# Linear attention in chunks of 64 tokens of two batches instead of 128 tokens of one

## The chip, the core and the metric

The kernel runs on one core of a Trainium2 chip. Five engines work side by side: TensorE (PE, with its weight loads shown apart as PEld), VectorE (DVE), ScalarE (ACT), GpSimd (POOL) and SyncE (SP), whose queue issues most of the transfers. They meet by semaphores only. The metric is the device time of one execution in microseconds (us), as the median of several runs.

## What is computed

Three layers follow one another: a linear attention with decay, a routed expert layer, and a dense layer with squared ReLU. The change touches only the first. In it, 4 batches of 8 heads with head dimension 48 run over 768 tokens; w (one decay per head and channel) scales the state from token to token, u weighs the token's own key and value.

```python
B, H, S, D = r.shape                       # 4, 8, 768, 48
for t in range(S):
    kt, vt, rt = (k[:, :, t], v[:, :, t], r[:, :, t])
    cur = np.einsum('bhd,bhe->bhde', u[None] * kt, vt)
    y[:, :, t] = np.einsum('bhd,bhde->bhe', rt, state + cur)
    state = w[None, :, :, None] * state + np.einsum('bhd,bhe->bhde', kt, vt)
```

The output rows (3072 tokens x 384) go to the router and the experts (`_moe_ref`), and then through `h = np.maximum(x @ w_in, 0.0)` and `(h * h) @ w_out` (`_moe2_ref`).

## The kernel before

The kernel is written out engine by engine; each engine's program order is fixed by hand, and semaphores release it.

**Units.** The attention is cut into 24 units (NU), six chunks of 128 tokens for each of four batches. Unit n = 4i + b is chunk i of batch b. Each batch has its own state tile, so a state that unit n leaves is needed again by unit n + 4. Heads go in four pairs (PAIRS): head a = 0 of a pair lies on partitions 0 to 47, head a = 1 on 64 to 111.

**One unit.** DVE scales keys and queries by powers of the decay (`scale`: `ks`, lines 710, and `rs`, 711). TensorE then runs these stages, of which each has a function:

- `scores` (L1166): 8 matmuls of keys against queries, weights 48 rows x 128 columns, 128 columns streamed, head 0 and head 1 by turns in the upper and lower rows of the array, into `sc_ps`, one bank for each.
- `inter` (L1179): 8 matmuls of queries against the state, weights 48 x 128, 128 columns streamed, into `y_ps`.
- `turn` (L1233): 3 transposes of the output rows of the unit before, 128 x 128.
- `back` (L1204): 16 matmuls of masked scores against values, weights 128 rows x 64 columns, 64 columns streamed, the two halves of the columns by turns, added to `y_ps`.
- `own_term` (L1220): 8 matmuls, weights 112 x 64, of which 2 columns are streamed (the term with u).
- `gate` (L1241): 6 matmuls, weights 128 x 64, 8 columns streamed (the router's logits of the unit before).
- `state_update` (L1192): 8 matmuls of scaled keys (`kn`) against values, weights 128 x 48, 48 columns streamed, into `u_ps`.

DVE masks the scores (`mask`, L717, two instructions of 128 x 512 from PSUM), adds the output's two parts (`rows`, L739) and updates the state (`state_sum`, L728, four instructions of 112 x 48). POOL makes `kn` (L426) and `rk` (L435) and splits a quarter of a dense weight tile (L441). ACT copies logits and transposed rows and scales values (L564). SP loads `tt` and `nn` four units ahead and stores the output rows (L334), one transfer of 128 rows for each unit.

**Order on TensorE.** In the loop's step for unit n it does scores(n+1), inter(n+1), turn(n-1), back(n), own_term(n+1), gate(n-1), state_update(n+1). DVE does mask(n+1), scale(n+2), rows(n), state_sum(n+1). `kn` and `u_ps` are single: `kn` of unit n+1 is made when state_update(n) is done, and `u_ps` is written again when state_sum(n) is done. The last chunk's units need no update; of them only unit 20 does one.

**Precision.** All matmuls of the attention are fp32. Each is recorded as two passes, with a weight load and a matmul for each pass; a transpose has one pass. So a stage of 8 matmuls has 16 records.

## Time and profile before

| | us |
|---|---|
| median of 3 runs | 809.96 |
| lowest, highest | 808.62, 810.9 |
| the profiled execution | 810.82 |
| its span in the trace | 809.1 |

The trace holds one execution. Its span begins with the first instruction and ends with the last; 1.7 us of the execution's own time lie around it. The attention fills the first 125 us or so, routing comes next, and the experts and the dense layer fill the rest. In the whole span PE is busy 775.9 us (96%), DVE 501.0 (62%), ACT 321.4 (40%), POOL 293.9 (36%). Starts of instructions are recorded; ends of matmuls are modelled, so lengths of stages are best read from one stage's start to the next one's.

### The profile page before, as it was taken

Reading aid. Unit: us, or ns where it says so; the run is one execution under the profiler, and the core shown is the slowest. Engines: PE = TensorE matmul, PEld = TensorE weight load, DVE = VectorE, ACT = ScalarE, POOL = GpSimd, SP = SyncE. Lnnn points to the kernel's source line nnn. Section 1 sums busy time; section 2 is a strip of 40 time slices with the busy share of each in tenths; the row PEclk is TensorE's granted clock in tenths of the full one; section 3 lists DMA queues with packets and bytes.
Section 4 is the critical chain, followed back from the end, with each engine's and each line's share of the span. In section 5 each row is a group of like instructions: output and inputs, shape, how many; then the busy total and the mean of one; then the engine's idle time right before and its main releaser. Section 6 shows DMA issues by size and latency. Waiting matters only on the chain.

```text
span 809.1 us, 19168 instructions
## 1 busy us (share of the span) xinstructions
PE 775.9 (96%) x6971; PEld 742.5 (92%) x6971; DVE 501.0 (62%) x1195; ACT 321.4 (40%) x718; POOL 293.9 (36%) x295
## 2 busy tenths in 40 slices
PE   8999994699999999999999999999999999999996
PEld 6999993589899999999999999999999999999995
DVE  7988886788846783678367836783778326721210
ACT  4566554314532354235323532353235324531432
POOL 7766640102631163116312631263126312621333
PEclk9999996799999999999999999999999999999998
DMA  8878744502300140014001400130013002300000
GB/s 225 260 236 244 240 122 176 184 2 79 108 1 30 35 149 0 29 42 142 0 29 49 135 0 29 52 133 0 29 59 126 0 30 79 108 1 30 0 1 30
DMA packets 22196, 65.27 MB, mean 81 GB/s; under 512 B 3664, under 2 KB 6736, under 8 KB 22160
## 3 DMA queue, kind: packets, MB, share of 16 engines
q1 hardware_dynamic: 19088, 55.34, 21.5%
q0 software_dynamic: 3072, 9.44, 3.3%
q8 instruction: 24, 0.39, 0.2%
q14 instruction: 12, 0.10, 0.0%
HBM read 55.33 MB, written 9.44 MB: 80 GB/s over the span
## 4 chain that ended last, share of the span: by engine, by line
PE 77%; DVE 12%; issue 5%; POOL 3%; ACT 1%; DMA 1%; POOLq 0%; DVEq 0%; SPq 0%; ACTq 0%
PE bank L1362 14%; PE bank L1372 13%; PE bank L1369 13%; PE bank L1429 6%; PE bank L1430 6%; PE bank L1431 6%; PE bank L1166 3%; PE bank L1204 3%; PE bank L1179 3%; DVE hot L977 2%; DVE sq L1076 2%; DVE w_lo L294 1%; PE bank L1233 1%; POOL xg L476 1%; PE bank L1220 1%
## 5 line engine op out<-in xcount | busy, mean ns | idle before, releaser
L503 POOL TENSOR_TENSOR h_lo<-sq,h_hi 128x384 fp32r<-128x384 f32 x128 | 155.4, 1217 | 376.2 <-DVE sq L1076 375.9
L1076 DVE SCALAR_TENSOR_TENSOR sq<-bank,relu 128x384 f32<-128x384 f32 x128 | 71.0, 555 | 150.7 <-ACT relu L627 148.7
L627 ACT ACTIVATE relu<-bank 128x384 f32<-128x384 f32 x128 | 62.8, 491 | 191.9 <-PE bank L1372 165.0
L1429 PE MATMUL bank<-m_hi,h_hi 128*128 128x384 f32 x384 | 132.5, 345 | 2.3 <-POOL h_lo L503 2.0
L1430 PE MATMUL bank<-m_lo,h_hi 128*128 128x384 f32 x384 | 130.0, 339 | 0.0
L1362 PE MATMUL bank<-x_hi,m_hi 128*128 128x384 f32 x384 | 129.6, 337 | 0.0
L1431 PE MATMUL bank<-m_hi,h_lo 128*128 128x384 f32 x384 | 129.6, 337 | 0.0
L1372 PE MATMUL bank<-x_hi,m_lo 128*128 128x384 f32 x360 | 121.6, 338 | 0.0
L1369 PE MATMUL bank<-x_lo,m_hi 128*128 128x384 f32 x360 | 121.0, 336 | 0.0
L621 ACT ACTIVATE h_hi<-bank 128x384 fp32r<-128x384 f32 x64 | 31.4, 491 | 175.3 <-PE bank L1372 149.4
L1068 DVE SCALAR_TENSOR_TENSOR h_lo<-bank,h_hi 128x384 fp32r<-128x384 f32 x64 | 35.5, 555 | 73.6 <-ACT h_hi L621 73.6
L1429 PEld LDWEIGHTS bank<-m_hi,h_hi 128*128 128x128 f32 x384 | 72.2, 188 | 4.5 <-POOL h_lo L503 4.5
L1362 PEld LDWEIGHTS bank<-x_hi,m_hi 128*128 128x128 f32 x384 | 72.4, 189 | 0.0
L1431 PEld LDWEIGHTS bank<-m_hi,h_lo 128*128 128x128 f32 x384 | 72.3, 188 | 0.0
L1430 PEld LDWEIGHTS bank<-m_lo,h_hi 128*128 128x128 f32 x384 | 72.3, 188 | 0.0
L629 ACT ACTIVATE h_hi<-relu 128x384 fp32r<-128x384 f32 x128 | 67.3, 526 | 4.1
L1372 PEld LDWEIGHTS bank<-x_hi,m_lo 128*128 128x128 f32 x360 | 67.9, 189 | 0.0
L1369 PEld LDWEIGHTS bank<-x_lo,m_hi 128*128 128x128 f32 x360 | 67.9, 189 | 0.0
L1362 PE MATMUL bank<-x_hi,w_hi 128*128 128x384 f32 x192 | 67.3, 351 | 0.0
L1362 PE MATMUL bank<-h_hi,w_hi 128*128 128x384 f32 x192 | 64.5, 336 | 1.9 <-DVE h_lo L1068 1.9
L294 DVE TENSOR_TENSOR w_lo<-w_raw,w_hi 128x1024 fp32r<-128x1024 f32 x48 | 63.9, 1335 | 2.1 <-ACT w_hi L597 2.1
L1372 PE MATMUL bank<-h_hi,w_lo 128*128 128x384 f32 x192 | 64.4, 336 | 0.0
(199 smaller groups left out, 1473.2 us busy)
## 6 DMA issues: line engine op xcount, KB each, us to landing
w_raw<-we_in SPq DMA_DIRECT2D x48, 512.0 KB
nn<-nn_in SPq DMA_DIRECT2D x24, 384.0 KB, 4.2
tt<-tt_in SPq DMA_DIRECT2D x44, 192.0 KB, 4.4
m_raw<-m_in SPq DMA_DIRECT2D x12, 512.0 KB, 6.4
x_rows<-yrow SPq DMA_DIRECT2D x24, 192.0 KB, 2.4
tt<-tt_in SPq DMA_DIRECT2D x4, 256.0 KB, 5.7
xg<-x_rows,perm_next POOLq DMA_INDIRECT x24, 5.1
out<-xg,perm_now POOLq DMA_INDIRECT x24, 2.6
```

Of the source, the lines that this page charges most:

```text
L294: eng.tensor_tensor(w_lo[:, cols], w_raw[j % W_SLOTS][:, :], w_hi[:, cols].bitcast(f32), ALU.subtract).then_inc(w_lo_ready, 1)
L503: pool.tensor_tensor(h_lo[g % 3][:, :], sq[g % 2][:, :], h_hi[g % 3][:, :].bitcast(f32), ALU.subtract).then_inc(lo2_ready, 1)
L627: act.activation(relu[:, :], h_ps[g % 3][:, 0:CAP], ACT.Relu).then_inc(relu_ready, 1)
L629: act.activation(h_hi[g % 3][:, :], relu[:, :], ACT.Square).then_inc(h_hi_ready, 1)
L1068: dve.scalar_tensor_tensor(out=h_lo[g % 3][:, :], in0=h_ps[g % 3][:, 0:CAP], scalar=0.0, in1=h_hi[g % 3][:, :].bitcast(f32), op0=ALU.max, ...
L1076: dve.scalar_tensor_tensor(out=sq[g % 2][:, :], in0=h_ps[g % 3][:, 0:CAP], scalar=0.0, in1=relu[:, :], op0=ALU.max, op1=ALU.mult).then_inc ...
L1362: pe.matmul(out, hi_w, hi_x, start=first, stop=False)
L1369: pe.matmul(out, hi_w, lo_x, start=False, stop=False)
L1372: return pe.matmul(out, lo_w, hi_x, start=False, stop=last)
L1429: pe.matmul(acc_ps[t][:, 0:DM], h_hi[r][:, s], m2_hi[:, c:c + DM], start=first, stop=False)
L1430: pe.matmul(acc_ps[t][:, 0:DM], h_hi[r][:, s], m2_lo[:, c:c + DM], start=False, stop=False)
L1431: last = pe.matmul(acc_ps[t][:, 0:DM], h_lo[r][:, s], m2_hi[:, c:c + DM], start=False, stop=end)
```

## The change

A unit becomes a chunk of 64 tokens of two batches: tokens 0 to 63 of a unit belong to the one batch (c = 0), 64 to 127 to the other (c = 1). There are still 24 units, now 12 chunks of 2 pairs of batches, and a state tile holds two batches side by side (112 x 2 x 48 x 4). A state that unit n leaves is needed again by unit n + 2. On the host the inputs are put into this order.

- `scores` and `inter` become 16 matmuls each, weights 48 x 64, 64 columns streamed, over all four 64x64 tiles of the array.
- `state_update` becomes 16 matmuls, weights 64 x 48, in two halves: `update_straight` (rows of batch c into the columns of head c) before `turn`, and `update_across` (the other two tiles), laid between the matmuls of `back`.
- `back` keeps 16 matmuls of 64 columns, with 64 rows in place of 128: only the two straight tiles.
- `mask` becomes one instruction of 128 x 512 for both heads; `state_sum` four of 112 x 96.
- The power tables have 64 columns in place of 128. ACT copies a corner of the causal mask early, and shifts half of the unit numbers late.
- The rows of a unit are stored by two transfers of 64 rows. Unit 21 does an update too.
- TensorE's waits for the stages now stand apart from the matmuls (`pe_held`), and `back` waits for `inter_done` and for `update_half` as well.

```diff
+C = 64
+NB = 2
@@
-                    sp.dma_start(x_d[bass.ds(i * P + b * S, P), :], yrow[b][:, :]).then_inc(y_stored[b], 16)
+                    for c in range(NB):
+                        sp.dma_start(x_d[bass.ds(i * P + b // NB * C + (b % NB * NB + c) * S, C), :],
+                                     yrow[b][c * C:(c + 1) * C, :]).then_inc(y_stored[b], 16)
@@ mask
-                for a in range(2):
-                    dve.tensor_tensor(am[b % 2][:, a, :].rearrange("p (c t) -> p c t", c=4),
-                                      sc_ps[a].rearrange("p (c t) -> p c t", c=4),
-                                      causal[:, :].unsqueeze(1).broadcast_to([P, 4, P]), ALU.mult).then_inc(masked, 1)
+                dve.tensor_tensor(am[b % 2][:, :, :, :], sc_ps.rearrange("p a (q t) -> p a q t", q=PAIRS),
+                                  causal[:, 0:C].unsqueeze(1).unsqueeze(2).broadcast_to([P, 2, PAIRS, C]), ALU.mult).then_inc(masked, 1)
@@ state_sum
-                    done = dve.scalar_tensor_tensor(out=state[b][:, c], in0=state[b][:, c], scalar=w_chunk[:, p:p + 1],
-                                                    in1=u_ps[0:HD, c], op0=ALU.mult, op1=ALU.add)
+                    done = dve.scalar_tensor_tensor(out=state[b % NB][:, :, c], in0=state[b % NB][:, :, c], scalar=w_chunk[:, p:p + 1],
+                                                    in1=u_ps[0:HD, :, c], op0=ALU.mult, op1=ALU.add)
@@ scores
-                        last = pe.matmul(sc_ps[a][:, p * P:(p + 1) * P], ks[rows, p, :], rs[j][rows, p, :], start=True, stop=True)
+                        for t in range(0, P, C):
+                            last = pe.matmul(sc_ps[t:t + C, a, p * C:(p + 1) * C], ks[rows, p, t:t + C], rs[j][rows, p, t:t + C],
+                                             start=True, stop=True)
@@ inter
-                        last = pe.matmul(y_ps[j][:, a, p * P:(p + 1) * P], rs[j][rows, p, :], state[b][rows, p * D:p * D + P],
-                                         start=p == 0, stop=False)
+                        for c in range(NB):
+                            t = slice(c * C, (c + 1) * C)
+                            last = pe.matmul(y_ps[j][t, a, p * P:p * P + C], rs[j][rows, p, t], state[b % NB][rows, c, p * D:p * D + C],
+                                             start=p == 0, stop=False)
@@ state_update
+            def update_tile(b, p, a, c):
+                h = slice((2 * p + a) * D, (2 * p + a + 1) * D)
+                t = slice(c * C, (c + 1) * C)
+                return pe.matmul(u_ps[a * HALF:a * HALF + D, c, p * D:(p + 1) * D], kn[t, h], nn[b][t, 0, h], start=True, stop=True)
+            def update_straight(i, b):
+                n = 4 * i + b
+                pe.wait_ge(kn_ready, n + 1)
+                if not is_first(n):
+                    pe.wait_ge(state_ready, n + B // NB)
+                pe.sem_inc(pe_held, 1)
+                for p in range(PAIRS):
+                    for c in range(NB):
+                        last = update_tile(b, p, c, c)
+                last.then_inc(update_half, 1)
+            def update_across(b, p):
+                for c in range(NB):
+                    last = update_tile(b, p, 1 - c, c)
+                return last
@@ back
+                def token_tile(p, a, c):
+                    t = slice(c * C, (c + 1) * C)
+                    at = (2 * p + a) * D
+                    return pe.matmul(y_ps[j][t, a, p * P:p * P + C], am[j][t, a, p, :],
+                                     nn[b][t, :, :].rearrange("p x f -> p (x f)")[:, at:at + C], start=False, stop=p == PAIRS - 1)
                 for p in range(PAIRS):
                     for a in range(2):
+                        if update is not None and a == 1:
+                            crossed = update_across(update[1], p)
+                            if p == PAIRS - 1:
+                                crossed.then_inc(update_ready, 1)
+                        for c in range(NB):
+                            last = token_tile(p, a, c)
@@ units of TensorE
+                    if more:
+                        update_straight(*one)
+                    turn(n - 1, (b - 1) % B)
+                    back(i, b, one if more else None)
```

TensorE's program in the steady part of the attention, before: one turn of the loop's stages, each row a line, what it writes and reads, the columns of the weights x the columns streamed, and the count.

```order
L1166 MATMUL bank<-rs,ks 128x128 x8
L1179 MATMUL bank<-state,rs 128x128 x8
L1233 MATMUL bank<-ident,yrow 128x128 x3
L1204 MATMUL bank<-nn,am 64x64 x16
L1220 MATMUL bank<-u_pair,rk 64x2 x8
L1241 MATMUL bank<-wg,yT 64x8 x6
L1192 MATMUL bank<-nn,kn 48x48 x8
```

TensorE's program at the same place after the change, from the end of one unit's `back` into the next unit's; L1184 is `scores`, L1201 `inter`, L1209 the update, L1294 `turn`, L1257 `back`, L1281 `own_term`, L1302 `gate`.

```order
L1209 MATMUL bank<-nn,kn 48x48 x2
L1257 MATMUL bank<-nn,am 64x64 x4
L1209 MATMUL bank<-nn,kn 48x48 x2
L1257 MATMUL bank<-nn,am 64x64 x2
L1281 MATMUL bank<-u_pair,rk 64x2 x8
L1302 MATMUL bank<-wg,yT 64x8 x6
L1184 MATMUL bank<-rs,ks 64x64 x16
L1201 MATMUL bank<-state,rs 64x64 x16
L1209 MATMUL bank<-nn,kn 48x48 x8
L1294 MATMUL bank<-ident,yrow 128x128 x3
L1257 MATMUL bank<-nn,am 64x64 x2
L1209 MATMUL bank<-nn,kn 48x48 x2
```

The update moved from the end of the unit to both sides of `turn`, and a unit has 81 matmuls where it had 57.

DVE's program in the loop, one unit, before and then after.

```order
L717 TENSOR_TENSOR am<-bank,causal 128x512 x2
L710 TENSOR_TENSOR ks<-tt,kpow 112x512
L711 TENSOR_TENSOR rs<-tt,powr 112x512
L739 TENSOR_TENSOR yrow<-bank,ownv 128x384
L728 SCALAR_TENSOR_TENSOR state<-state,w_chunk,bank 112x48 x4
```

After the change, the same place:

```order
L734 TENSOR_TENSOR am<-bank,causal 128x512
L728 TENSOR_TENSOR ks<-tt,kpow 112x512
L729 TENSOR_TENSOR rs<-tt,powr 112x512
L755 TENSOR_TENSOR yrow<-bank,ownv 128x384
L744 SCALAR_TENSOR_TENSOR state<-state,w_chunk,bank 112x2x48 x4
```

The order of DVE's steps stays; one mask instruction is gone, and the four of the state are twice as wide.

## Rows read from the trace of the kernel before

**Rows 1.** Busy time by engine, stretches of the attention; columns as in its first line.

```profile
core 0: us, PE busy (x) PEld busy (x) DVE busy (x) ACT busy (x) POOL busy (x), PEclk, DMA share, GB/s
20.00:40.00 20.00, 19.96 (x481) 18.49 (x480) 18.43 (x37) 11.87 (x46) 16.11 (x15) 1.00 0.85 258
...
80.00:100.00 20.00, 20.00 (x466) 18.49 (x462) 17.44 (x39) 12.53 (x50) 13.69 (x14) 1.00 0.79 236
20.00:108.00 88.00, 87.96 (x2083) 81.55 (x2084) 78.78 (x168) 52.25 (x207) 60.30 (x58) 1.00 0.81 242
```

**Rows 2.** Waits from 20 to 108 us, longest first.

```profile
engine line waited for: us in total, times, longest us
ACT own L552 <- PE bank L1241: 26.5, 19, 1.5
POOL kn L426 <- PE bank L1192: 23.3, 17, 1.9
...
DVE am L717 <- PE bank L1166: 5.2, 17, 0.3
PEld bank L1204 <- issue: 3.2, 19, 0.2
...
DVE state L728 <- PE bank L1192: 2.3, 4, 0.6
...
PEld bank L1166 <- DVE rs L711: 0.2, 1, 0.2
```

**Rows 3.** Timeline of TensorE, one unit: start, length, engine, line, operation, operands, weights, shape, records.

```profile
start us, us, engine line op out<-in xcount [idle before <-releaser]
...
93.34 1.16 PE L1166 MATMUL bank<-rs,ks 48*128 48x128 f32 x16
94.34 1.06 PE L1179 MATMUL bank<-state,rs 48*128 48x128 f32 x16
95.33 0.55 PE L1233 MATMUL bank<-ident,yrow 128*128 128x128 f32 x3
95.81 1.15 PE L1204 MATMUL bank<-nn,am 128*64 128x64 f32 x32
96.79 0.58 PE L1220 MATMUL bank<-u_pair,rk 112*64 112x2 f32 x16
97.23 0.50 PE L1241 MATMUL bank<-wg,yT 128*64 128x8 f32 x12
97.58 0.54 PE L1192 MATMUL bank<-nn,kn 128*48 128x48 f32 x16
98.05 0.38 PE L1166 MATMUL bank<-rs,ks 48*128 48x128 f32 x2
```

**Rows 4.** Chain of work that ended last, the same stretch.

```profile
19 pieces in order of time: start us, us, what
...
97.73 0.39 PE bank L1192 x16
98.12 1.09 PE bank L1166 x16
99.21 0.89 PE bank L1179 x16
```

**Rows 5.** Timeline in windows of some ns: first weight loads and matmuls of one `scores`.

```profile
93.34 0.19 PEld L1166 LDWEIGHTS bank<-rs,ks 48*128 48x128 f32 x2
...
93.45 0.19 PEld L1166 LDWEIGHTS bank<-rs,ks 48*128 48x128 f32 x2
...
93.34 0.38 PE L1166 MATMUL bank<-rs,ks 48*128 48x128 f32 x2
...
93.34 0.48 PE L1166 MATMUL bank<-rs,ks 48*128 48x128 f32 x3
```

**Rows 6.** DVE's groups from 20 to 108 us.

```profile
line engine op names shapes xcount | busy us, mean ns | idle before us <-releasers
L717 DVE TENSOR_TENSOR am<-bank,causal 128x512 f32<-128x512 f32 x36 | 23.2, 686 | 5.3 <-PE bank L1166 5.2
L710 DVE TENSOR_TENSOR ks<-tt,kpow 112x512 f32<-112x512 f32 x19 | 19.2, 1009 | 0.0
L711 DVE TENSOR_TENSOR rs<-tt,powr 112x512 f32<-112x512 f32 x19 | 16.1, 850 | 0.0
L728 DVE SCALAR_TENSOR_TENSOR state<-state,w_chunk,bank 112x48 f32<-112x48 f32 x75 | 14.8, 259 | 3.6 <-PE bank L1192 2.3
L739 DVE TENSOR_TENSOR yrow<-bank,ownv 128x384 f32<-128x384 f32 x19 | 10.4, 548 | 0.3
```

**Rows 7.** Timeline of POOL in that unit.

```profile
93.50 1.00 POOL L426 TENSOR_TENSOR kn<-nn,kpow_n 128x384 f32<-128x384 f32 x1 [0.65 <-PE bank L1192]
```

**Rows 8.** Timeline of the attention's start.

```profile
12.52 1.00 POOL L426 TENSOR_TENSOR kn<-nn,kpow_n 128x384 f32<-128x384 f32 x1 [1.76 <-DVE kpow_n L703]
...
13.23 1.06 PE L1179 MATMUL bank<-state,rs 48*128 48x128 f32 x16
...
14.83 0.79 DVE L728 SCALAR_TENSOR_TENSOR state<-state,w_chunk,bank 112x48 f32<-112x48 f32 x4
...
15.54 0.96 DVE L710 TENSOR_TENSOR ks<-tt,kpow 112x512 f32<-112x512 f32 x1
...
16.42 0.68 DVE L711 TENSOR_TENSOR rs<-tt,powr 112x512 f32<-112x512 f32 x1
...
17.15 0.97 PEld L1166 LDWEIGHTS bank<-rs,ks 48*128 48x128 f32 x16 [0.71 <-DVE rs L711]
```

**Rows 9.** Transfers issued from 60 to 80 us: KB each, us to landing.

```profile
tt<-tt_in SPq DMA_DIRECT2D x8, 192.0 KB, 4.2
x_rows<-yrow SPq DMA_DIRECT2D x5, 192.0 KB, 2.4
```

More of the change, by code:

```diff
@@ L222, in build @@
         bank = [banks[:, j, :] for j in range(8)]
-        sc_ps, y_ps, tr_ps, u_ps = bank[0:2], [banks[:, 2 + 2 * j:4 + 2 * j, :] for j in range(2)], bank[6], bank[7]
+        sc_ps, y_ps, tr_ps = banks[:, 0:2, 0:PAIRS * C], [banks[:, 2 + 2 * j:4 + 2 * j, :] for j in range(2)], bank[6]
+        u_ps = bank[7][:, 0:NB * PAIRS * D].rearrange("p (c f) -> p c f", c=NB)
         lg_ps, own_ps = tr_ps[:, 504:512], tr_ps[:, 496:504]
@@ L365, in _ @@
             sp.wait_ge(logit_ready, NU)
+            for b in range(B):
+                sp.wait_ge(y_stored[b], 16 * NB * (NC + 1))
             load_expert(0)
@@ L378, in _ @@
             pool.memset(causal[:, :], 1.0).then_inc(made, 1)
-            for b in range(B):
-                pool.memset(state[b][:, :], 0.0).then_inc(state_ready, 1)
+            for m in range(B // NB):
+                pool.memset(state[m][:, :, :], 0.0).then_inc(state_ready, 1)
             pool.wait_ge(made, 3)
@@ L444, in units @@
                 for b in range(B):
-                    if not last:
+                    if not last or b == 0:
                         updates(i + (b + 1) // B, (b + 1) % B)
@@ L760, in units @@
                     rows(i, b)
-                    if not last:
+                    if not last or b == 0:
                         state_sum(*one)
@@ new lines, in may_cross, with state_update, back @@
+            def may_cross(i, b):
+                pe.wait_ge(update_half, 4 * i + b + 1)
+                pe.sem_inc(pe_held, 1)
+            def state_update(i, b):
+                may_cross(i, b)
+                for p in range(PAIRS):
+                    last = update_across(b, p)
+                last.then_inc(update_ready, 1)
+            def back(i, b, update=None):
+                n, j = 4 * i + b, b % 2
+                pe.wait_ge(masked, n + 1)
+                pe.wait_ge(inter_done, n + 1)
+                pe.wait_ge(nn_in[b], 16 * i + 16)
+                if update is None:
+                    pe.sem_inc(pe_held, 1)
+                else:
+                    may_cross(*update)
+                def token_tile(p, a, c):
[3 more added lines that the diff above has]
+                                     nn[b][t, :, :].rearrange("p x f -> p (x f)")[:, at:at + C], start=False, stop=p == PAIRS - 1)
```

101 lines of the change are left out of this document (49 added, 52 removed).

## The prediction

> **What bounds the kernel now.** I began with the busy time by stretches. From 20 to 108 us TensorE is busy 87.96 of 88.00 us at a granted clock of 1.00, and DVE 78.78 [rows 1]. The list of waits says the same: the other engines wait for TensorE (ACT 26.5 us, POOL 23.3), while TensorE's own rows come to 3.2 us of issue, which lie on its weight loads, and a single 0.2 us on DVE [rows 2]. So in the attention TensorE is the bound, and DVE, busy for 90%, stands close behind it. What the change is worth is the new length of one unit on TensorE, times some 20 units, unless DVE is then longer.
>
> One unit, by the starts of its stages [rows 3]: scores 1.00 us, inter 0.99, turn 0.48, back 0.98, own term 0.44, gate 0.35, update 0.47; sum 4.71, and the next unit's scores begin at 98.05, 4.71 after 93.34.
>
> **What paces one matmul.** This decides the case. The own term streams 2 columns and the gate 8, next to nothing, and yet they take 0.44/8 = 0.055 and 0.35/6 = 0.058 us a matmul [rows 3]. Back streams 64 columns and takes 0.98/16 = 0.061, its first one included. What these have in common is 64 columns of weights in two passes. The update with 48 columns of weights takes 0.39 us for 8, the first one's load included, so 0.043 to 0.049 each; inter with 128 columns takes 0.89 for 8, 0.111 each [rows 4]. The time goes with the columns of the weights and not with the columns streamed: one load after the other, about 0.058 us for 64 columns, 0.046 for 48, 0.112 for 128. Before this change no stage is held by streaming alone; the tiles do stream side by side, and this hides the stream behind the loads.
>
> Do loads of different tiles run side by side? The start of scores shows it. Just there the array is empty, and the second matmul goes to other rows of it. In the window up to 93.44 only the first matmul's two loads have started; the second one's start at 93.45, 0.11 later. The first two matmul records start at 93.34, a third only by 93.56, when the second load is through [rows 5]. So the load of another tile, with nothing in its way but the first load, waited for it. The alternation of own term and gate between the two column halves shows the same for these. I take it that four tiles load one after another too. The nearest row for a 64x64 tile is back's, 0.058.
>
> **TensorE, stage by stage.** Scores: 16 x 0.058 = 0.93, and 0.05 for a first load that nothing covers, 0.98 (was 1.00). Inter: 16 x 0.058 = 0.93 (was 0.99, of which 0.10 went, beyond 8 x 0.112, before the turn could begin; that gap now lies behind the straight update). Straight update: 8 x 0.046 = 0.37, and 0.10 for that gap, 0.47. Turn: 0.48 as now. Back with the update across between its matmuls: 16 x 0.058 + 0.05 + 8 x 0.046 = 1.35 (was 0.98). Then comes a gap that isn't there now: back and own term have today the same 64-column tiles with all rows, and afterwards the tile size changes between them. The row for such a change is inter's 0.10; bounds 0 and 0.20; I take 0.10. Own term 0.44. Gate 0.35, and 0.10 for the change of tile that today stands in the update's 0.47 (0.47 - 8 x 0.046). Sum: 0.98 + 0.93 + 0.47 + 0.48 + 1.35 + 0.10 + 0.44 + 0.45 = 5.20 us a unit, against 4.71: **0.49 us more**. Nearly all of it is the update, which has twice the loads (16 instead of 8, +0.37); scores and inter have twice the loads at half the width, which gives back only the fixed part.
>
> **Is TensorE still the bound?** DVE loses one mask (0.69) and its four state instructions grow from 48 to 96 columns: from 0.26 each to between 0.26 (a fixed cost) and 0.52 (by columns). Yrow with 384 columns takes 0.55, so 48 more columns cost (0.55 - 0.26)/7 = 0.04; I take 0.30. By means it is 0.69 + 1.01 + 0.85 + 0.55 + 4 x 0.30 = 4.29 [rows 6]. The same sum for before is 4.83, where busy time gives 78.78/88 x 4.71 = 4.22 [rows 1], since neighbours overlap; the factor 0.87 makes it 3.8 us. Under 5.20 that is covered. POOL's kn takes 1.00 [rows 7] and is now wanted before turn; between the end of the update across and the next straight update lie own term, gate, scores and inter, 2.8 us. Straight update also waits for the state sum of the unit before it, 0.55 + 1.2 us of DVE behind back, under the same 2.8. The dependence on the state of two units ago, four before, is longer than that. These cost nothing; if TensorE's unit were under 4.2 they would begin to. Behind a waiting straight update stand turn and back, and behind these DVE's yrow and SP's store.
>
> SP issues one store more a unit. The store of 192 KB lands in 2.4 us and the loads are issued four units ahead [rows 9]; nothing waits for either in the rows, so 0, and at most 2.4 us once at the end, where the gathers wait for the last store. ACT's two small additions stand where ACT waits; 0.
>
> **The two ends.** At the start TensorE waits for DVE: scores of unit 2 begin at 17.15, released by rs. In DVE's order the state sum stands ahead of that scaling. It starts at 14.83 today [rows 8]. Afterwards the straight update waits for kn, ready at 13.5, then inter and the update across follow (0.37 + 0.93 + 0.37, and two gaps), so the state sum starts near 15.3, takes 1.0, and 0.96 + 0.68 of scaling lead to 18.0. The lighter setup of POOL (two memsets for four) gives some 0.25 back: +0.6, between -0.4 and +1.2. At the end, unit 21 does an update that it didn't before: +1.0 with its gaps; unit 22 +0.2.
>
> **Sum.** Units 2 to 20: 19 x 0.49 = 9.3. With 0.6 + 1.0 + 0.2 it is +11.1. Routing and experts aren't touched. The profiled execution took 810.82, so it would take 821.9; the median stands 0.9 below it (809.96), so the forecast is **821.0 us**. The bounds of the terms: spacing of a 64-column load 0.055 to 0.061 on the 32 matmuls of scores and inter and the 16 of back (-0.14 to +0.14 a unit), the new gap 0 to 0.20, the update's load 0.043 to 0.049; together -0.2 to +0.2 a unit or 4 us in all, and about one at the ends. Own range 815 to 827.
>
> **Rival 1: loads of tiles in different rows run side by side (faster).** Then scores, inter and back with both updates need about half of their loads, TensorE's unit falls by some 1.7 to near 3.5, and DVE is the bound. DVE's 3.8 and two handovers, of which DVE's wait for scores today shows one (5.2 us in 17 waits, 0.3 [rows 2]), give 4.1 a unit, that is -0.6 on 20 units, and +0.6 at the start: 798. It decides from the point where a unit falls below 4.71: 48 loads at 0.058 and 16 at 0.046 are 3.5 us, so they must become 14% cheaper. For it speaks that the rows show row-tiled loads only in pairs of 128 columns. Against it speaks the second load of scores [rows 5], which had every chance to start. The Trainium skill, in TensorEngine Tiling, Key Properties, says that different tiles can execute LdWeights and Matmul in parallel. By that rule the change would end at rival 1. The trace agrees for the matmuls, and for the loads it doesn't, by the 0.11 us between the first two.
>
> **Rival 2: two row tiles that write one bank take turns (slower still).** Today heads 0 and 1 write separate banks. Straight update, update across and back now have tiles of different rows that write different partitions of one bank at the same time; no row shows that. A matmul of 128 columns holds its tile until the third record may start, 0.21 us [rows 5], so 64 columns hold it 0.107 and 48 some 0.08. Taking turns, back would cost 16 x (0.107 - 0.058) = 0.78 more and the straight update 8 x (0.080 - 0.046) = 0.27; the update across could fill the gaps. +1.05 on 20 units: 842. The Trainium skill, in TensorEngine Tiling, Gotcha 1, states that different row tiles cannot access the same PSUM bank simultaneously. If it means the whole bank, whatever the partitions, this rival is what comes; nothing in the trace before can tell.
>
> **Rival 3: loads overlap a little.** If only the second pass's load, or part of one, slips under another tile's, the unit comes out near today's: 806 to 814.
>
> **Chances.** Forecast 0.70, rival 1 0.20, rival 2 0.06, rival 3 0.04. Differences under 0.3% (2.4 us, about what a measurement of this kernel can tell) count as the same: 0.04 from rival 3. Faster 0.20, slower 0.70 + 0.06 = 0.76. The range that holds 8 in 10: the forecast's own 815 to 827 with a margin of 2 above, rival 3, and half of rival 1, so 800 to 829.
>
> **What the profile after would show.** Right: TensorE still busy for all of 20 to 108 us and a unit of about 5.2 us; scores and inter of 0.93 to 0.98 from start to start; back with its crossings 1.35; DVE's waits for TensorE longer, its busy share down to three quarters. Wrong by rival 1: scores and inter at half, TensorE's waits for DVE (rs, state, yrow) at the top of the list, a unit near 4.1. Wrong by rival 2: back near 2.1 us and the straight update near 0.75, scores and inter unchanged. Wrong at the gap: own term's start more than 0.2 after back's last matmul would be due. Wrong at the start: scores of unit 2 not near 18.

## The result and the profile after

| | before | changed |
|---|---|---|
| first chip, median of 9 runs | 812.17 us (808.62 to 820.18) | 821.71 us (816.64 to 861.07) |
| second chip, median of 11 and 8 runs | 811.42 us (809.03 to 812.15) | 817.25 us (812.23 to 822.62) |
| ratio, first chip | | 1.0086 (1.0044 to 1.0127) |
| ratio, second chip | | 1.0079 (1.0046 to 1.0112) |
| span of the profiled execution, mean granted clock | 809.1 us, 0.979 | 815.2 us, 0.956 (second chip) |

The forecast was 821.0 us and slower, and it came out so. The reason it gave is wrong all the same, and what follows is mostly about that. Medians are over all executions; each ratio is to the kernel before, run on the same chip, and leaves out the executions more than 1.5% above the fastest of their kernel (four of the changed kernel's nine on the first chip, whose other five have the median 818.71 us). The first profiled execution of the changed kernel spent 157 us in a row at the half clock and took 861 us, so the profile read here is the second chip's, of 816.96 us.

One unit of the attention on TensorE at full clock, in the timeline (columns as in [rows 3]):

```profile
90.48 0.69 PE L1184 MATMUL bank<-rs,ks 48*64 48x64 f32 x32
91.00 0.65 PE L1201 MATMUL bank<-state,rs 48*64 48x64 f32 x32
91.48 0.56 PE L1209 MATMUL bank<-nn,kn 64*48 64x48 f32 x16
91.98 0.55 PE L1294 MATMUL bank<-ident,yrow 128*128 128x128 f32 x3
92.45 0.27 PE L1257 MATMUL bank<-nn,am 64*64 64x64 f32 x2
...
93.53 0.63 PE L1281 MATMUL bank<-u_pair,rk 112*64 112x2 f32 x16
94.02 0.50 PE L1302 MATMUL bank<-wg,yT 128*64 128x8 f32 x12
94.45 0.29 PE L1184 MATMUL bank<-rs,ks 48*64 48x64 f32 x4
```

Start to start: scores 0.52 us (forecast 0.98), inter 0.48 (0.93), straight update 0.50 (0.47), turn 0.47 (0.48), back with the update across 1.08 (1.35, and 0.10 for a gap), own term 0.49 (0.44), gate 0.43 (0.45). The sum is 3.97 us, against 4.71 before [rows 3] and 5.20 forecast. So at full clock the changed unit is **0.74 us shorter**, though it has 81 matmuls for 57.

VectorE at the same time:

```profile
89.89 0.54 DVE L755 TENSOR_TENSOR yrow<-bank,ownv 128x384 f32<-128x384 f32 x1
90.36 0.98 DVE L744 SCALAR_TENSOR_TENSOR state<-state,w_chunk,bank 112x96 f32<-112x96 f32 x4
91.26 0.68 DVE L734 TENSOR_TENSOR am<-bank,causal 128x512 f32<-128x512 f32 x1
```

It has no idle time in these rows either; from one `yrow` to the next it takes 3.8 to 3.9 us. The mask takes 0.68 in one instruction (two of them before, [rows 6]) and the four state instructions 0.98 in all. Both engines are now near the bound.

Where did the gain go? First the whole stretch that the prediction looked at, then its parts: busy time and granted clock by stretches (PE's columns are those of [rows 1]):

```profile
20.00:108.00 88.00, 82.99 (x2800) 75.99 (x2800) 64.62 (x142) 48.16 (x194) 56.21 (x54) 0.83 0.76 219
...
6.40:13.20 6.80, 4.84 (x130) 3.76 (x128) 5.54 (x11) 1.75 (x8) 4.96 (x20) 1.00 1.06 248
13.20:26.90 13.70, 11.36 (x275) 10.71 (x275) 7.17 (x15) 3.99 (x13) 7.71 (x8) 0.50 0.82 235
26.90:37.10 10.20, 8.29 (x324) 7.47 (x320) 7.68 (x16) 5.00 (x22) 6.38 (x6) 1.00 0.71 195
37.10:43.90 6.80, 6.80 (x163) 6.33 (x159) 3.34 (x8) 3.56 (x12) 3.00 (x3) 0.50 0.68 176
...
47.40:64.40 17.00, 17.00 (x381) 15.34 (x379) 7.62 (x19) 5.76 (x23) 6.34 (x7) 0.50 0.69 196
64.40:124.00 59.60, 56.26 (x2222) 51.49 (x2224) 52.46 (x113) 39.81 (x159) 44.81 (x42) 1.00 0.82 238
```

The seventh value is the clock: 0.50 (1.2 GHz) for 13.7 + 6.8 + 17.0 = 37.5 us of the first 64, where before it was 1.00 (2.4 GHz) from 4.5 to 127 us. At half clock a unit takes 6.89 us (in the first chip's profile 15 units in a row do). By the starts of scores, unit 9 begins at 65.17 us for 50.66 before, 14.5 us late; from there to unit 23 it takes 58.7 us for 65.6, so 6.8 us come back. Routing and experts give 1.6 more, and 6.1 us remain. The whole loss lies in the first nine units.

In them TensorE also stops three times without a wait (three places of the timeline, then its waits):

```profile
15.00 0.77 PE L1209 MATMUL bank<-nn,kn 64*48 64x48 f32 x14
17.79 1.12 PE L1257 MATMUL bank<-nn,am 64*64 64x64 f32 x17 [2.02 <-issue]
...
34.19 0.28 PE L1257 MATMUL bank<-nn,am 64*64 64x64 f32 x4
36.38 0.27 PE L1257 MATMUL bank<-nn,am 64*64 64x64 f32 x2 [1.91 <-issue]
...
45.43 0.22 PE L1201 MATMUL bank<-state,rs 48*64 48x64 f32 x1
46.47 0.63 PE L1201 MATMUL bank<-state,rs 48*64 48x64 f32 x28 [0.82 <-issue]
```

The second and the third stop stand inside a row of matmuls of one line, where no semaphore is waited for. Counted in order of time through all of TensorE's records in the trace, 449 stand ahead of the first stop, 1473 ahead of the second and 1985 ahead of the third: 4 x 256 and 2 x 256 apart. The trace has transfers on a queue that it calls "q8 instruction" (28 packets and 0.46 MB in the execution, so 16384 bytes each, which is 256 times 64). They start at 15.1, 19.5, 24.3, 28.8, 33.6, 37.8, 43.6, 49.1, 52.8, 56.7 and 63.6 us, last 0.9 to 1.5 us each, and the next comes at 116.5 us: none in the loop's further rounds, and again with the last round, which is written out behind the loop. That they are TensorE's I take from where it stops. When those of 15.1 and 33.6 us landed, TensorE stood at the 256-boundary already; it went on 1.3 to 1.4 us later. It went on just as long after the one of 43.6 us had landed. Before, a unit has 54 x 4 + 3 x 2 = 222 instructions (a load and a matmul for each of two passes) in 4.71 us, 47 per us; now 78 x 4 + 6 = 318 in 3.97, 80 per us. From this came **theory S**: code that runs for the first time is supplied in blocks, the changed kernel eats it faster than it comes, TensorE stops, and the stops bring the clock down.

The time of an execution follows the clock. Over the 17 executions of the changed kernel on both chips, the time at half clock (2 x (1 - mean clock) x span) goes from 52 to 184 us, and the span is 790.7 us + 0.367 x that time, with a correlation of 0.98. The long executions carry much of this: over the 13 that the ratios use it is 801.0 us + 0.217 x, with a correlation of 0.76. Before mostly has 32 to 40 us of it, in its profile all of them behind the attention.

### The profile page after: what moved, and what is told of

Read it like the earlier page. It is cut to its first block, busy times and chain, and to the rows that moved or that the text cites. A ratio compares the mean times of both kernels' runs of the same rounds, so it can differ in the third digit from the quotient of the medians.

```text
span 859.3 us, 21520 instructions
## 1 busy us (share of the span) xinstructions
PE 821.4 (96%) x8107; PEld 782.9 (91%) x8107; DVE 484.4 (56%) x1175; ACT 322.5 (38%) x720; POOL 291.2 (34%) x294
## 4 chain that ended last, share of the span: by engine, by line
PE 86%; DVE 6%; issue 3%; DMA 1%; POOL 1%; ACT 1%; SPq 0%; POOLq 0%; DVEq 0%; ACTq 0%
PE bank L1430 15%; PE bank L1440 14%; PE bank L1437 13%; PE bank L1497 7%; PE bank L1498 7%; PE bank L1499 7%; PE bank L1257 5%; PE bank L1184 3%; PE bank L1281 2%; PE bank L1294 2%; PE bank L1201 2%; PE bank L1209 2%; PE bank L1302 2%; PE bank L1436 1%; PE bank L1432 1%
```

## Experiments

**e1_after_again**: the changed kernel again, with no edit, on the second chip.

> The changed kernel unaltered, for more profiles of it. Theory A (loads of tiles in different rows run side by side, so that a unit needs less of TensorE, but TensorE's clock is granted at half for a part of the attention that differs from run to run): at a granted clock of 1.00 scores and inter take about 0.5 us each from start to start and a unit 4.1 to 4.5, at 0.50 scores 0.9 and a unit 6.9; the time goes with the share of the attention at half clock, 816 to 835 us. Theory B (the sum of the prediction, one load after another at full clock): scores and inter take 0.93 to 0.98 at a granted clock of 1.00 and a unit 5.2.

Measured: 817.25 us, ratio 1.0079 (1.0046 to 1.0112). It is the run shown above.

**e4_pairs**: what does one matmul of a tile cost? The kernel before, with blocks of 16 fp32 matmuls of `ident` into a free part of `y_ps`, one kind of tile and of turn each.

```diff
                 pe.wait_ge(state_ready, n + 1)
+                if isinstance(n, int):
+                    tile_tests(n - 1)
```

> The kernel before with blocks of 16 extra fp32 matmuls ahead of six of its inter stages (full clock), each block with another pair of tiles; their results are cleared by inter. 2 columns streamed, so that weight loads set the pace: all rows with the column halves by turns (L1174), one 64x64 tile (L1176), same 64 rows with column halves by turns (L1180), row halves by turns in the same columns (L1183), the two straight tiles (L1187), all four tiles (L1190), row halves with 128 columns (L1194). 64 columns streamed: the two straight tiles into two banks (L1197), the same into one bank (L1201), one tile (L1204), four tiles (L1207). Theory B (loads one after another everywhere): L1174 to L1190 all 0.058 us a matmul, 0.93 a block, L1194 0.112, L1207 0.058. Theory A: 0.058 for tiles that share rows (L1174, L1176, L1180), about 0.03 for L1183, L1187, L1190 and L1207, 0.06 for L1194. Rival on banks: L1201 0.107 against 0.058 for L1197; otherwise they are alike. L1204: 0.107 to 0.11 either way, the stream of one tile.

Measured: 838.92 us (one run). The blocks that ran at full clock, by their first and last record (32 records, two a matmul):

```profile
L1204 PE MATMUL bank<-ident x32: 218/218/268, 143.4 to 145.2; 64*64 64x64 f32 x32
L1201 PE MATMUL bank<-ident x32: 218/218/267, 137.8 to 138.7; 64*64 64x64 f32 x32
L1207 PE MATMUL bank<-ident x32: 218/218/267, 145.2 to 145.7; 64*64 64x64 f32 x32
L1176 PE MATMUL bank<-ident x32: 193/194/215, 19.5 to 21.3; 64*64 64x2 f32 x32
L1194 PE MATMUL bank<-ident x32: 168/248/248, 128.9 to 130.5; 64*128 64x2 f32 x32
```

L1204 stays on one 64x64 tile: 1.8 us, 0.117 a matmul. L1201 takes turns between the two diagonal tiles: 0.9, 0.058. L1207 goes round all four: 0.47, 0.030 (by the trace's ns). L1176 stays on one tile and streams only 2 columns: 0.117 again, where theory A had 0.058. So a matmul in two passes costs its tile 0.117 us, and **four tiles work at once, with their loads**. The 0.058 that the prediction read as the price of one 64-column load was two tiles overlapping; L1194, two row halves with 128 columns of weights, takes 0.104 to 0.112, and one alone 0.224 (below). The Trainium skill, TensorEngine Tiling (Array Packing), Key Properties, says that different tiles can execute LdWeights and Matmul in parallel; this run agrees, 0.117 against 0.030. L1201 also settles rival 2: its tiles of different rows write different partitions of one bank, at 0.058, with no turn taken. Gotcha 1 of the same page of the Trainium skill (different row tiles cannot access the same bank simultaneously) doesn't hold for different partitions here.

How do two tiles look at their first loads? Weight loads in the first hundredths of a microsecond of L1204 (one tile) and of L1201 (two):

```profile
143.37 0.13 PEld L1204 LDWEIGHTS bank<-ident 64*64 64x64 f32 x1
...
137.78 0.14 PEld L1201 LDWEIGHTS bank<-ident 64*64 64x64 f32 x2
```

One tile alone starts one load, and its second pass's load comes 0.05 us later; two tiles start two loads within 0.01 us. The first `scores` of the kernel before had two loads at 93.34 and two more at 93.45 [rows 5]. The trace doesn't say which tile a load belongs to, but by this pattern the pair is one load of each tile, and the 0.11 us is each tile's wait for its own first pass. Then [rows 5] showed the overlap already.

The same run bears on the clock, which the next experiments are about:

```profile
17.70:21.50 3.80, 3.79 (x78) 1.00 1.05 304
21.50:38.60 17.10, 17.10 (x234) 0.50 0.38 108
```

This is the kernel before, and from 17.2 to 130 us TensorE has no idle time of 0.1 us. All the same the clock fell at 21.5 us, at the end of the two blocks that stream 2 columns (L1174 and L1176, 3.2 us), and likewise at 41.9 and 130.7 us, in or right behind the others of 2 columns (L1187 with L1190, and L1194). Behind the three of 64 columns from 137.8 to 145.8 us it stayed full until 154.6. So it falls without any stop too.

**e2_fill2, e3_fill6**: more dense work in each unit against the half clock, 2 and 6 bf16 matmuls of 256 columns.

```diff
                 pe.sem_inc(pe_held, 1)
+                if not (isinstance(n, int) and n < 1):
+                    fill(2, j)
```

> The changed kernel with two bf16 matmuls of 128x128 weights and 256 columns (0.11 us each at full clock) ahead of every inter from unit 1 on, into a bank that inter then clears; nothing else is changed. Theory A: if the clock falls for lack of dense work, these keep it at 1.00 for more of the attention, and the time falls to between 797 and 812 us although TensorE does more work. Theory B, and any theory in which the clock isn't the taker: 24 x 0.22 = 5 us more than the changed kernel.

> The same with six such matmuls a unit, 0.64 us at full clock. Theory A: the clock stays at 1.00 for all of the attention; TensorE's unit is then about 4.4 to 4.6 us, near the unit of the kernel before, and the time 800 to 808 us. Theory B: 24 x 0.64 = 15 us more than the changed kernel, 832 or more.

Measured: 827.73 us, ratio 1.0202 (1.0184 to 1.0220), and 833.14 us, 1.0263 (1.0213 to 1.0313). Neither clears the half clock: it is 0.50 for 27.4 us from 59.6 us on in the one, for 10.2 us from 64.0 us on in the other. A unit at full clock is 4.41 and 4.84 us, and TensorE stops for up to 2.4 us in both, at the same 449 + 256 k records as before. The fills come with instructions of their own. Theory A's times are missed by both; e3_fill6 falls where theory B had it (832 or more), e2_fill2 some 5 us above it, and B's loads one after another are refuted by the units all the same. As a cure both miss.

**e5_short_loads, e6_before_short**: do the data's transfers hold up the instructions'?

```diff
-                        load_tt(b, 4 * i + b + 4)
+                        load_tt(b, 4 * i + b + 4, 8)
...
-                        load_nn(b, 4 * i + b + 4)
+                        load_nn(b, 4 * i + b + 4, 16)
```

> The changed kernel with the loads of tt (16 of 112 partitions) and nn (16 of 128) cut short from unit 4 on; their values are stale, so this run leaves out part of the inputs, and all waits and engine instructions stay. Theory S (supply): TensorE's halts of 0.8 to 2.2 us at 16384-byte places of its instruction stream (17.8, 36.4, 46.5 us in the undisturbed profile of the changed kernel) come from instruction packets that queue behind the data's in the DMA engines (76% busy up to 100 us), and the half clock from 13 to 64 us follows from the halts. Then halts shrink to under 0.3 us each, the clock stays full from about 20 us on, 20 units take about 4.15 us each, and the run takes 795 to 802 us. Theory F (fixed cadence): instruction blocks come one in 4 to 5 us whatever the other queues do; halts, half clock and time stay, 814 to 818 us. Theory M: halts go but the clock stays half in the same stretches, 810 to 814 us.

> The kernel before with the same short loads of tt and nn from unit 4 on (stale inputs, the same waits): the control for e5_short_loads. Theories S, F and M all expect what the trace of before shows: TensorE asks for 222 instructions per 4.7 us, no halt in its stream, clock full up to 127 us, units limited by TensorE. So 809 to 813 us, within 0.3% of before. If it gains over 3 us, the loads cost something else than instruction supply and the reading of e5_short_loads has to allow for it.

Measured: e5_short_loads 814.01 us, ratio to before 0.9988 (0.9939 to 1.0036); e6_before_short 811.27 us, 0.9989 (0.9958 to 1.0021). For e5_short_loads, the stretches and the waits of TensorE from 17 to 60 us:

```profile
26.40:53.70 27.30, 23.76 (x935) 1.00 0.32 85
53.70:64.00 10.30, 10.30 (x224) 0.50 0.22 55
```

```profile
PE bank L1257 <- issue: 3.1, 2, 2.3
PE bank L1209 <- issue: 1.7, 2, 0.9
PE bank L1302 <- issue: 0.6, 1, 0.6
...
```

With 85 GB/s of traffic for 195 the instruction packets come evenly: from 24.4 to 56.0 us nine of them, one in 3.95 us on average (3.5 to 4.1), 65 instructions per us. From 35 us on TensorE stops at **every** boundary, 0.4 to 0.95 us each, and five units from 28.0 to 52.3 us take 4.86 us each on a full clock: 318 / 4.86 = 65 per us. That is the supply. So theory F was right that there is a cadence which stays when the loads go. With the loads the intervals are 3.7 to 6.9 us; part of that is the half clock, under which a unit asks for 318 instructions in 6.89 us only. I had expected S's form, with the stops gone, and it missed. But F's time missed too: set against the kernel before on the same chip, the run is at 0.9988 where the changed kernel is at 1.0079, some 7 us better. The loads don't make the stops, yet without them the stops behind 20 us are under 1 us and the full clock holds for 27.3 us. The clock held through four such stops and fell behind the fifth. e6_before_short doesn't move: before is short neither of loads nor of instructions.

**e12_many_small**: more instructions than the supply, in the kernel before.

```diff
                 pe.wait_ge(state_ready, n + 1)
+                if isinstance(n, int) and 2 <= n <= 4:
+                    for m in range(64):
+                        r, t = m // 2 % 2 * 64, m % 2 * 64
+                        pe.matmul(y_ps[j][t:t + 64, r // 64, 0:64], ident[r:r + 64, 0:64], ident[r:r + 64, 0:64], start=True, stop=True)
```

> The kernel before with a block of 64 more fp32 matmuls in 64x64 tiles of all four quarters (256 TensorE instructions) ahead of inter in units 2, 3 and 4, and nothing else. By the 0.030 us of such a matmul each block takes 1.9 us if instructions are there, so 5.7 us are added. Theory S (supply, one block of 16384 bytes in 4.0 us or slower, whatever the kernel): inside or behind the blocks TensorE halts at places 256 instructions apart, 1 to 2.5 us each and 2 to 6 us in all, with no wait that the profile names, the clock falls to half behind them, and the run takes 819 to 830 us. If the halts belong to the changed kernel's own order and not to the number of instructions: no such halts, full clock to about 130 us, 816 to 818 us.

Measured: 826.53 us, ratio 1.0179 (1.0141 to 1.0217). Timeline at the second block, and the waits from 20 to 60 us:

```profile
29.41 1.16 PE L1183 MATMUL bank<-state,rs 48*128 48x128 f32 x15
32.36 0.27 PE L1183 MATMUL bank<-state,rs 48*128 48x128 f32 x1 [1.80 <-issue]
```

```profile
PE bank L1183 <- issue: 3.6, 2, 1.8
PE bank L1208 <- issue: 1.6, 1, 1.6
```

The stops (1.85, 1.80 and 1.59 us) stand inside `inter` and `back` of the old form, behind 705, 1217 and 1729 records of TensorE, on the same grid 449 + 256 k as in the changed kernel. The number of new instructions makes the stops, not the change's order. After the third the clock was 0.50 for 10.2 us, after the first two it stayed. The sum closes: 809.1 us, 3 x 2.03 for the blocks, 5.2 of stops and, as an estimate from the unit's two lengths, some 4.5 for the half clock make 824.9; the span is 825.8.

**e9_halts_in_before**: stops without any new instructions; ScalarE clears 16 x 128 columns of `hot` once more and then raises `halt`.

```diff
                         gate(n - 1)
+                        if isinstance(n, int) and n < 4:
+                            pe.wait_ge(halt, n)
```

> The kernel before, with TensorE halted three times in its first units: after the gate of units 1, 2 and 3 it waits for a ScalarE activation of 16 x 128 columns (about 1.9 us with its start-up, by the 2.76 us for 24 x 128). Three halts of about 2.2 us between 22 and 40 us, 6 to 7 us in all; no 64x64 tile form and no more instructions than before. Theory S (halts bring the clock down): the granted clock falls to 0.50 within some us of a halt and stays there for 10 to 30 us, and a unit there takes about 8 us, so 821 to 833 us. Theory T (the many small tiles bring it down, not the halts): the clock stays 1.00 from 4.5 to about 130 us and only the halts are added, 816 to 819 us.

Measured: 825.63 us, ratio 1.0130 (1.0085 to 1.0175). Stretches, and the wait:

```profile
23.90:30.70 6.80, 6.60 (x75) 0.50 0.63 163
30.70:34.10 3.40, 1.25 (x44) 1.00 0.36 84
34.10:40.90 6.80, 6.80 (x79) 0.50 0.35 105
```

```profile
PE bank L1195 <- ACT hot L581: 6.4, 3, 2.1
```

The three stops end at 24.1, 34.1 and 44.2 us, and with each end the clock is at 0.50 for 6.8 us, 20.5 us in all; then it stays full to 143 us. They cost 6.4 us themselves and some 9 through the clock (824.7 - 809.1 - 6.4). A stop of 2.1 us alone brings the clock down, so theory T isn't needed for it; that other things bring it down as well e4_pairs has shown. The old form is back at 1.00 after 6.8 us each time here, but in e4_pairs only after 13.7 us from 41.9 us on, with its ordinary stages alone from 42.5 us. The changed one is back after 6.8 to 17 us, with e8_in_high_early's edit once after 34, and in one run after 157.

**e11_fill_first**: fills in the first units alone.

```diff
                 pe.sem_inc(pe_held, 1)
+                if isinstance(n, int) and 1 <= n <= 4:
+                    fill(12, j)
```

> The changed kernel with 12 bf16 fill matmuls of 256 columns (about 0.11 us each) ahead of inter in units 1 to 4 alone. They lengthen those units by 1.3 us and bring the demand there to about 342 instructions in 5.3 us, 64 per us. Theory S: no or short halts up to 40 us, the two first stretches at half clock (13.2 to 26.9 and 37.1 to 43.9 us) go or shrink by 10 us or more; 5.2 us are added and 5 to 9 us come back: within 4 us of the changed kernel, and the mean granted clock rises by 0.01. If halts and half clock stay as they are, 5 us are lost: 821 to 826 us.

Measured: 831.06 us, ratio 1.0227 (1.0141 to 1.0312).

```profile
17.30:41.20 23.90, 21.11 (x662) 1.00 0.66 182
41.20:51.40 10.20, 9.94 (x225) 0.50 0.51 150
```

As S wants, slower eating removed the stop at 17.8 us, the only other one on the grid before 41 us is 0.44 us, and the clock is full from 17.3 to 41.2 us. Then come the units without fills, stops of 2.1 and 2.2 us (ahead of 41.5 and 57.0 us), and half clock behind both. So the link of stop and clock holds here too. But the fills are also dense work of their own, and this run can't tell whether the full clock comes from them or from the missing stops. The expected time (within 4 us of the changed kernel) is missed: the cure costs more than it returns.

**e7_wide_own_gate**: fewer instructions, meant to cost no time.

```diff
-                    for t in range(0, P, HALF):
-                        last = pe.matmul(own_ps[t:t + HALF, 2 * p:2 * p + 2], rk[j][:, p, t:t + HALF], u_pair[:, p, :],
-                                         start=True, stop=True)
+                    last = pe.matmul(own_ps[:, 2 * p:2 * p + 2], rk[j][:, p, :], u_pair[:, p, :], start=True, stop=True)
...
+                    last = pe.matmul(lg_ps, yT[:, d * P:(d + 1) * P], wg[:, d, :], start=d == 0, stop=d == DC - 1)
```

> The changed kernel with own term and gate in 128-column weight tiles: 4 and 3 matmuls in place of 8 and 6, the same TensorE time by the measured 0.112 us for 128 columns against 2 x 0.058, but 28 instructions fewer in each unit (about 290 in place of 318). Theory S: demand falls from 80 to 73 instructions per us against a supply of one block of 256 in 4 to 5 us, so halts get shorter and fewer and less of attention runs at half clock: 2 to 10 us faster than the changed kernel on the same chip (807 to 815 us). Theory F+ (clock independent of the halts) and a TensorE that is limited by its own work: within 1.5 us of the changed kernel, 815.5 to 818.5.

Measured: 849.84 us, ratio 1.0412 (1.0301 to 1.0523).

```profile
116.65 1.05 PE L1280 MATMUL bank<-u_pair,rk 112*128 112x2 f32 x8
117.56 0.81 PE L1299 MATMUL bank<-wg,yT 128*128 128x8 f32 x6
```

```profile
78.30:88.50 10.20, 10.20 (x191) 0.50 0.79 225
88.50:91.90 3.40, 3.40 (x107) 0.99 0.23 55
91.90:102.10 10.20, 10.20 (x182) 0.50 0.60 174
```

The run misses as a test, and shows the error of the prediction in another place. The own term takes 0.91 us for 0.49 and the gate 0.75 for 0.43 (the next `scores` begin at 118.31): a 128-column load costs 0.112 *a pass*, 0.224 a matmul, and two 64-column tiles side by side cost half of that. My 0.112 "for 128 columns" had come from inter, two row halves overlapping. That is 0.74 us a unit, 15 us. Of half clock this run has 112 us, some of it from 78 to 102 us, where TensorE is busy all the time and no instruction packet comes. **So stops are not the only thing that holds the clock down.** What holds it there I can't say from these runs. It fits e4_pairs that own term and gate, with 2 and 8 columns streamed, now fill 1.66 of a unit's 4.67 us and filled 0.92 of 3.97; that wasn't tested.

**e10_bf16_scores**: fewer instructions by less precision; it leaves out the fp32 of scores and inter.

```diff
-        rs = [sb(f"rs{j}", [HD, PAIRS, P], f32, att) for j in range(2)]
-        ks = sb("ks", [HD, PAIRS, P], f32, att)
+        rs = [sb(f"rs{j}", [HD, 2, PAIRS, P], bf16, att)[:, 0, :, :] for j in range(2)]
+        ks = sb("ks", [HD, 2, PAIRS, P], bf16, att)[:, 0, :, :]
...
+        state = [sb(f"state{m}", [HD, 2, NB, PAIRS * D + C - D], bf16, att)[:, 0, :, :] for m in range(B // NB)]
```

> The changed kernel with rs, ks and the states stored in bf16, so that scores and inter are bf16 matmuls of one pass: it leaves out the fp32 precision of these, and each unit has 64 TensorE instructions fewer (about 254 in place of 318) and about 0.5 us less TensorE work; VectorE's work is the same or less. Theory S (supply): at 3.93 us per unit the demand is 65 instructions per us, about the 64 per us of the fetches, so halts are under 0.5 us each, the clock stays full from about 27 us on, and the run takes 797 to 806 us. Theory L (less work on TensorE brings the clock down by itself): halts shrink as well, but the clock is half for as long as in the changed kernel or longer, also after 66 us, 812 to 825 us.

Measured: 819.46 us, ratio 1.0087 (1.0071 to 1.0104).

```profile
85.50:88.90 3.40, 3.25 (x65) 0.50 0.87 270
88.90:102.60 13.70, 11.82 (x441) 1.00 0.87 247
102.60:106.00 3.40, 3.21 (x88) 0.50 0.88 276
```

```profile
PE bank L1210 <- DVE state L745: 2.5, 8, 0.4
PE bank L1282 <- issue: 1.9, 2, 0.9
```

The stop at 22.6 us is 4.2 us long; from 24 to 60 us those on the grid are shorter (0.6, 1.6 and 0.5 us), and a full-clock unit is 3.8 us. TensorE now waits for VectorE in it, so VectorE is the bound as soon as TensorE has less to do. But the clock falls in the steady part as well, at 85.5 and 102.6 us, where there is no supply stop and TensorE is busy 0.86 of the time; 91 to 112 us at half clock in each execution. The two idle times of the second row, 0.95 and 0.93 us, end 1.5 and 1.1 us before these falls; they are the gap in every fourth unit that the next experiment explains. In the changed kernel the same gap is 0.7 to 1.0 us, and no fall follows within 3 us. Theory L's time came true. Whether less work or the longer gap brings the clock down isn't separated. Taking work off TensorE alone would therefore not have brought the gain.

**e8_in_high_early**: the gap in every fourth unit, in which ScalarE splits a dense weight tile ahead of the copy that the own term waits for.

```diff
                         turned_y(n - 1)
+                        if not last and b == B - 1:
+                            in_high(i + 1)
                         act.wait_ge(logit_sum, n)
...
-                    if not last and b == B - 1:
-                        in_high(i + 1)
```

> The changed kernel with ScalarE's split of m_raw (1.04 us, once in four units) moved from behind own_values to the idle 1.2 to 1.5 us ahead of own_copy. Theory: in every fourth unit at full clock (4.78 us against 3.93 us) the own term waits for the copy behind that split; moved, the 0.85 us goes in each of the two to four units of that kind that run at full clock: 1.5 to 3.5 us faster than the changed kernel, about 814 us. Rival: the 0.7 to 1.0 us idle ahead of the own term has another holder (instruction supply at the loop's end); then nothing changes, 816 to 818 us.

In the changed kernel every fourth unit at full clock is 4.78 us; its waits from 20 to 116 us have this row, and those of e8_in_high_early from 60 us on have no such row:

```profile
PE bank L1281 <- issue: 2.3, 3, 0.8
```

Measured: all units from 85 to 101 us take 3.92 to 3.97 us, so the mechanism is right: ScalarE's 1.04 us split stood ahead of the copy that the own term needs. The unit after them takes 5.20 us, with TensorE waiting 1.2 us for VectorE's `rs`, so a part of what was gained is lost to the next bound. The time is 823.59 us all the same, ratio 1.0126 (1.0087 to 1.0164): stops of 3.1 and 2.2 us, and 34 us at half clock after the second. Its ten executions fit 788.0 us + 0.385 x the time at half clock (67 to 173 us). Against the changed kernel's line that is 1.4 us less at 70 us of half clock and nothing at 150, within the scatter of the points: a gain in time isn't shown.

## Why the prediction came out, point by point

- **TensorE bounds, DVE close behind**: right before the change; after it both are at 3.9 us, and e10_bf16_scores shows DVE taking over.
- **"One load after the other"**: this step failed. It rests on reading the two loads at 93.34 [rows 5] as both passes of one matmul, so that the other tile's load seemed to wait 0.11 us. In e4_pairs a tile alone starts one load and its next 0.05 us later, and two tiles start two loads at once; so the pair was most likely one load of each tile. And the 0.058 per 64 columns, from stages in which two tiles alternate, was taken for the price of one load. I took two tiles side by side for one in a queue. e4_pairs gives 0.117 for a tile alone and 0.030 for four; scores and inter came to 0.52 and 0.48, not 0.98 and 0.93, back with its crossings to 1.08, not 1.35 + 0.10. The unit was due at 5.20 and takes 3.97, every fourth 4.78, on average 4.10 (11 units in 45.09 us).
- **Rival 1** (loads overlap, 4.1 a unit, 798 us) had the right mechanism and nearly the right unit, with a chance of 0.20. Its sum fails because it counts no supply of instructions and no clock, and the waits for DVE that it set at the top of TensorE's list didn't come: what stands there is issue. As an estimate, with supply and clock in order, units 2 to 9 at 4.2 us from 17.8 us on would put unit 9 at 47 us instead of 65, and the span at 797.
- **The other terms**: no turns on a bank (rival 2 is out, e4_pairs). The gaps between tile sizes show as own term 0.49 and gate 0.43 in the place of 0.44 and 0.35, 0.13 for 0.20. DVE's unit was put at 3.8 and is 3.8 to 3.9. ScalarE's cover was put at nothing to pay; under a unit of 4.2 it began to cost 0.8 in every fourth. Scores of unit 2 were due at 18.0 and came at 21.65, with a stop of 2.02 and a clock at half from 13.2 us.
- **The number**: +11.1 forecast from +0.49 in each of 19 units; +6 to +10 measured, which is made of other things: for the second chip's profile, -0.6 us in each of 21 units (-12.8), three stops (+4.7), 37.5 us at half clock (37.5 x (1 - 4.0/6.89) = +15.7) and -1.6 behind the attention: +6.0 against the 6.1 of the spans. This is an estimate, as the first stop lies in a stretch at half clock and part of it is counted twice. The agreement is luck, and the profile's own check, "TensorE busy for all of 20 to 108 us and a unit of about 5.2 us", refutes the reason: it is busy 82.99 of 88.00 us. DVE's busy share of that stretch did go down to the three quarters that were forecast (64.62 of 88.00), but by the half clock and the stops; from 64.4 to 108 us, at full clock, it is 88%.

Shown: the overlap of tiles (e4_pairs), the supply and its grid (e5_short_loads, e12_many_small), that a stop of 2.1 us lowers the clock (e9_halts_in_before), and that blocks of 2 streamed columns do so with no stop (e4_pairs). Argued only: that the queue's packets are TensorE's, and that in the changed kernel the stops cause its half clock, rather than the kind of its matmuls; nothing removed the stops and left the rest alone. Open: why the clock stays at half so long in the changed form and falls in e7_wide_own_gate and e10_bf16_scores without a supply stop; and the first fall at 13.2 us, behind idle times of 0.3 to 0.9 us at the start. No version here beats the kernel before. One would have to run more of the attention in code that has been fetched already, a shorter first pass and loop; that wasn't tried.

## What to carry to other kernels

Before a spacing between matmuls is read as the price of a resource, take one tile alone and all tiles in turn: two that take turns look like one at half the price. When a change halves the work of an instruction and doubles their number, divide instructions by time in the code's first pass, and look for stops marked "issue" at even distances in the program. And price the granted clock with the rest: a gain of 0.7 us a unit was worth less than nothing here. A stop of 2 us mostly took the clock down for what followed (in e12_many_small 1.85 and 1.80 us didn't and 1.59 us did), and so did stretches of work that stream 2 columns.

## What the runs showed of the hardware

- TensorE's new code came in blocks of 16384 bytes, where it waited for them on average one in 3.95 us (e5_short_loads): 65 instructions per us. The stops up to 66 us that no wait explains stand at 449 + 256 k records in all ten traces that have them. The loop's later rounds, from 64 to 116 us, needed none. The Trainium skill, Trainium Architecture — The Big Picture, The software stack, has 64-byte instructions, which are moved into each engine at load. By that size a block holds 256 of them, and the distance of the stops agrees; that all blocks are there from the start isn't so here, as 28 come during the run.
- An fp32 matmul on a 64x64 tile holds it for 0.117 us with 2 or with 64 columns streamed; four tiles overlap fully, to 0.030.
- The granted clock fell with stops of 2.1 us (e9_halts_in_before) and, without a stop, behind blocks of 2 streamed columns (e4_pairs, at 21.5, 41.9 and 130.7 us). It stood at 0.50 with TensorE busy for 17.00 of 17.00 us in the changed kernel. The Trainium skill, TensorE: Matmul & The Clock Gate, Part 1, has the clock set by how busy the engine has been. The stops agree with that; the stretches at half clock with no idle time are not explained by it if every matmul of the trace counts as busy.
